# Two feed-forward layers on one core: the moving operands of the matmuls are read in another order

## What is computed

```python
# attention over channels: q, k, v are (1, 6016, 256)
qn = q / (norm(q, axis=1) + 1e-6)
kn = k / (norm(k, axis=1) + 1e-6)
a = softmax(kn.T @ qn / tau)          # 256 x 256, sum + 1e-9
x = v @ a                             # 6016 x 256
# layer 1
h = x @ w_in1                         # 6016 x 2048
y = where(h > 0, h, exp(min(h, 0)) - 1) @ w_out1
# layer 2
h = y @ w_in2
out = (h / (1 + exp(-h))) @ w_out2
```

## Time and profile before

| | |
|---|---|
| median of 3 runs | 1125.82 us (1121.5 to 1126.94) |
| profiled execution, its own time | 1125.11 us |
| its span in the profile | 1123.3 us |
| granted TensorE clock, mean | 0.998 |
| busy: PE / PEld / DVE / ACT | 99% / 82% / 58% / 39% |
| first stage, up to the first matmul of line 672 | 56 us |
| phases | about 68 us to the end |

### The profile page before, as it was taken

One profiled execution on the slowest core, in us unless ns is written; L12 is line 12 of the kernel. 1 busy time (PEld: TensorE's weight loads), 2 busy tenths in 40 slices (PEclk: granted clock), 3 DMA queues, 4 the chain that ended last, 5 costly groups with the idle time before them and its releaser, 6 DMA issues.

```text
span 1123.3 us, 14121 instructions
## 1 busy us (share of the span) xinstructions
PE 1116.8 (99%) x4944; PEld 916.1 (82%) x4944; DVE 647.8 (58%) x1106; ACT 439.8 (39%) x729; POOL 0.8 (0%) x7
## 2 busy tenths in 40 slices
PE   9899999999999999999999999999999999999999
PEld 8788888888888888888888888888888888889888
DVE  6698754654655564464465465465456446447444
ACT  5565542442443343343343244244233334334321
POOL 0000000000000000000000000000000000000000
PEclk9999999999999999999999999999999999999999
DMA  8833101101101010010110110110100001001001
GB/s 293 259 113 94 38 1 19 19 0 19 19 0 19 0 19 10 9 19 0 19 19 0 19 19 0 19 19 0 19 3 15 14 0 19 1 1 20 1 1 33
DMA packets 108039, 33.34 MB, mean 30 GB/s; under 512 B 95856, under 2 KB 100592, under 8 KB 108016
## 3 DMA queue, kind: packets, MB, share of 16 engines
q1 hardware_dynamic: 108016, 33.04, 12.1%
HBM read 26.87 MB, written 6.16 MB: 29 GB/s over the span
## 4 chain that ended last, share of the span: by engine, by line
PE 99%; DMA 1%; DVE 0%; ACT 0%; issue 0%; SPq 0%; POOL 0%; DVEq 0%; POOLq 0%
PE bank L672 93%; PE bank L683 3%; PE bank L770 2%; DMA early_qk<-k 1%; PE bank L703 0%; DVE early_square_sums L538 0%; PE bank L692 0%; ACT early_squares L448 0%; DVE early_scores L579 0%; PE bank L696 0%; ACT early_scores L467 0%; PE bank L714 0%; DVE small L582 0%; DVE out_tile L661 0%; SPq L355 0%
## 5 line engine op out<-in xcount | busy, mean ns | idle before, releaser
L672 PE MATMUL bank<-g_parts,w_out_parts 128*128 128x512 f32 (+1 forms) x2208 | 569.6, 393 | 0.0
L672 PEld LDWEIGHTS bank<-g_parts,w_out_parts 128*128 128x128 f32 x2208 | 413.9, 188 | 95.5
L620 DVE TENSOR_TENSOR g_parts<-g_raw,g_parts 128x512 fp32r<-128x512 f32 (+1 forms) x384 | 262.1, 682 | 50.9 <-ACT g_parts L488 30.4
L672 PE MATMUL bank<-y1T_parts,w_in_parts 128*128 128x512 f32 x1056 | 275.0, 395 | 0.0
L672 PE MATMUL bank<-vT_parts,a_w_in 128*128 128x512 f32 (+1 forms) x1056 | 269.2, 390 | 0.0
L513 ACT ACTIVATE g_raw<-bank 128x512 f32<-128x512 f32 (+1 forms) x192 | 113.0, 588 | 345.1 <-PE bank L672 337.6
L672 PEld LDWEIGHTS bank<-y1T_parts,w_in_parts 128*128 128x128 f32 x1056 | 198.3, 188 | 47.6
L672 PEld LDWEIGHTS bank<-vT_parts,a_w_in 128*128 128x128 f32 x1056 | 197.4, 188 | 44.1
L640 DVE CAST g_parts<-g_raw 128x512 fp32r<-128x512 f32 (+1 forms) x192 | 80.8, 421 | 240.5 <-ACT g_raw L513 240.4
L510 ACT ACTIVATE exp_h<-bank 128x512 f32<-128x512 f32 (+1 forms) x192 | 112.9, 588 | 263.0 <-PE bank L672 262.9
L633 DVE TENSOR_SCALAR exp_h<-exp_h 128x512 f32<-128x512 f32 (+1 forms) x192 | 80.7, 421 | 157.8 <-ACT exp_h L510 157.7
(11 more groups left out here) (62 smaller groups left out, 254.4 us busy)
## 6 DMA issues: line engine op xcount, KB each, us to landing
early_qk<-q SPq DMA_DIRECT2D x23, 256.0 KB, 3.4
early_qk<-k SPq DMA_DIRECT2D x23, 256.0 KB, 4.3
out<-out_tile SPq DMA_DIRECT2D x45, 128.0 KB, 2.6
v_in<-v SPq DMA_DIRECT2D x44, 128.0 KB, 3.1
early_w_in<-w_in SPq DMA_DIRECT2D x2, 1024.0 KB, 8.0
early_w_out<-w_out SPq DMA_DIRECT2D x2, 1024.0 KB, 10.8
weight_stage<-w_in SPq DMA_DIRECT2D x4, 512.0 KB, 5.8
weight_stage<-w_out SPq DMA_DIRECT2D x4, 512.0 KB, 3.9
```

Source lines behind the costliest of these rows:

```text
L620: dve.tensor_tensor(part(1), g_sb[:, f % 2, 0:ph.n], part(0).bitcast(F32), ALU.subtract).then_inc(u_lo, 1)
L672: mm = pe.matmul(dst, lhsT, rhs, start=first and n == 0, stop=last and n == len(todo) - 1)
```

## The change

Two helpers describe the same words in another order. For a tile of 512, `by_turns` reads words 0, 256, 1, 257, 2, 258, ... of a partition, and `evens_then_odds` reads 0, 2, 4, ..., 510, 1, 3, ..., 511. In `up` the moving operand is read `by_turns`, in every phase but the last, so column 2j of h belongs to token j of the tile and column 2j + 1 to token 256 + j. In `down` g is read `evens_then_odds`, which puts the columns of y back in the order of the tokens. In a tile of 384 the halves are 192 words.

```diff
+        by_turns = lambda x: x.rearrange("p (a b) -> p b a", a=2)
+
+        evens_then_odds = lambda x: x.rearrange("p (b a) -> p a b", a=2)
...
+                streamed = (lambda x: x) if ph is PH[-1] else by_turns
                 product(h_ps[f % N_H][:, 0:ph.n],
                         [(lambda x, c=c: w[:, x, c, f * P:(f + 1) * P],
-                          lambda x, c=c: ph.x[:, x, c, 0:ph.n]) for c in range(CB)]).then_inc(u_up, 1)
+                          lambda x, c=c: streamed(ph.x[:, x, c, 0:ph.n])) for c in range(CB)]).then_inc(u_up, 1)
...
-                                   lambda x: gp[:, f % N_H, x, 0:ph.n])], f == 0, f == FB - 1)
+                                   lambda x: evens_then_odds(gp[:, f % N_H, x, 0:ph.n]))], f == 0, f == FB - 1)
```

## The result

The changed kernel takes 1569.2 us (median, 1568.81 to 1570.64) against 1125.37 us in the same comparison: a ratio of 1.3953, with a 95% interval of 1.3917 to 1.399. The forecast was 1547, in a range of 1120 to 1970. The number is close, and it is close for the wrong reason: the kind of product that was to double its time became faster, and the kind that was to stay as it was doubled.

What follows compares the result with a forecast made beforehand. TensorE's unbroken matmul stream was taken to bound the kernel. To the profiled 1125.11 us came +421 us for first products at two cycles a column and 0 for second products: 1547 us, in a range of 1120 to 1970.

Steps and rivals of the forecast that it cites:

- What bounds the kernel: TensorE's matmuls of line 672, one unbroken chain of 1034.51 us; the end moves one for one with their pace.
- Step (1): All engines: no instruction, wait or transfer added, removed or moved; the same 4944 matmuls; priced at zero.
- Step (2): Changed matmuls: 2112 first products of 512 columns and 96 of 384, and as many second products.
- Step (3): First products in `up`, read alternately from two halves: two cycles a column, 426 ns per 512-column matmul, +421 us.
- Step (4): Second products in `down`, even columns first: neighbours remain near, taken as 0, with bounds of -42 and +421 us.
- faster: Rival, 13%: contiguous reading causes the 20 ns above 213 on changed matmuls; 1038 us, or 1082 with first products alone.
- Both kinds halve: Rival, 11%: a fetch is two words wide, so second products waste half of it too; +842, 1967 us.
- The test named beforehand: Six first products 2.56 us, six second 1.40; wrong if first pace moves under 10 ns or second more.

Runs made afterwards that it cites:

- the first kernel: First products in `up` read by turns, `down` left as it was, against the kernel before the change: 1086.33 us against 1124.43, ratio 0.9681.
- the slot with every word twice: One of 16 reading orders in the second executed trace: words 0, 0, 1, 1, 2, 2 in tiles of 512; 216 ns a matmul.
- the ladders: Three kernels, each giving the 16 slots (first and second product pairs) of a phase their own reading order; executed once each: 1281.22, 1141.21 and 1568.9 us.

## Why the prediction came out, point by point

**What bounds the kernel: right.** The end moved by the pace of TensorE's matmuls one for one; the chain stayed one piece and ScalarE's waits absorbed the difference. Reading the pace from starts, and not from means of overlapping records, was what made every later reading possible.

**Step (1), nothing else moves: right.** Same instructions, same counts, VectorE and ScalarE as busy as before, clock at 1.00.

**Step (2), the counts: right**, shown by the first kernel's 39 us from 352 groups of six.

**Step (3), first products at two cycles a column, +421 us: wrong in sign.** They became faster, 233 to 215 ns where nothing slow stands beside them, -38 us. The sentence that failed is "Alternation between two distant places separates every pair of neighbours". It took the stream for one reader. The runs show what fits two, one for the even places and one for the odd; by turns, each of them walks through neighbours, better than in place.

**Step (4), even columns first, 0: wrong.** The expected cost of the other step lay here: 450 ns, +482 us alone. "A fetch of four words still gives two used ones" is true of the stream and, by the picture of two readers, false of each, which uses one. The doubt was put at the right place (how wide a fetch is), but not its cause: the line is four words wide, as assumed, and the loss came all the same.

**The size** "two cycles a column" (426 ns) was read from the fp32 passes of line 683 and was 24 ns too small against 450; it fits 256 stays of 1.77 ns better than half the array's rate. One figure beside the sum is off as well and changes nothing: 2.4 words per ns are 2.5 times VectorE's one word in 1.04 ns, not 2.3.

**The total** was near since the two kinds of product have the same counts, so that a doubling costs the same on either side: +421 forecast, +482 - 38 = +444 measured. That is luck. Of the rivals, "faster" had the first products right in that the contiguous reading itself costs, with a floor of 213 ns against 216 measured; its example, near words that queue for one bank, does not fit the slot with every word twice, at 216. Its argument against, that a good part of the excess is per matmul, held only for the 2.5 ns that are left, of 20; its own figures, 12, 15 and 20 ns for 256, 384 and 512 columns, grow with the columns. "Both kinds halve" had the right price for the second ones. No case had one of each sign, the combination that came.

**The test named beforehand** caught it: six first products at 2.56 us "if right" were at 1.33, six second ones at 1.40 "if (4) is right" were at 2.70. By the prediction's own last sentence it is wrong: the second products' pace, which was to stay within 10 ns, moved by 217. Of the pages weighed, the Trainium skill, "SBUF — State Buffer", Specifications (TRN2), names lines of 16 bytes and two hits for full bandwidth. Applied to the stream, it gave both terms wrong; applied to even and odd places apart, the ladders agree with its line and nearly with its two hits (two give 233 ns, three give 215). The Trainium skill, "Vector Engine (DVE) Microarchitecture Reference", section 5.2, says that on VectorE a single read stream that alternated between two regions ran at the full rate; for TensorE the kernel with the first products alone agrees, with 215 ns.

## What to carry to other kernels

For a moving operand of four-byte words, look at every second column of the stream: that walk, and the one of the columns between, should find three or four of its words in each line of 16 bytes, and start on a line. Reading by turns from two places at least four words apart does that and was worth 7% here. One walk with a step of two words or more at every column is the expensive one (at two words it took 450 ns instead of 233), and an order that is awkward to undo can be undone in the copy out of PSUM, where steps of up to four words cost nothing to ScalarE. A total that fits does not confirm its terms: one part alone, in two kernels, showed at once that both were wrong.

## What the runs showed of the hardware

- The moving stream behaves as if fetched by two readers in turn, each keeping two lines of 16 bytes and not four: 216 ns for 512 columns at four words a stay, 215 for 510 columns at three, 233 for 512 at two, 431 to 527 at one (453 with even words first). "Two readers" is inferred from 48 slots of orders and not seen in any record.
- Reading in place, the plainest order, is not the fastest: it sits at two words a stay and loses 17 ns of 233. The lines' borders show as well: fours by turns over 504 columns cost 230 two words later instead of 213, and 266 one word later. In place, the start made no such difference (230 to 233).
- A matmul that wrote pairs of words to two halves of its PSUM bank in turn was not slower than one that wrote them side by side in the same order of reading (327 against 344 ns).
- Left open: 280 ns for four places in turn, 344 for pairs, 250 for fours from two halves, the spread from 431 to 527 at one word a stay, and why reading in place takes 233 where 128 stays of 1.77 ns make 227.
